# The first expert slot computed among the last attention tiles

## What is computed

```python
a = softmax(where(is_sink | in_window, q @ k.T / 8, -1e9));  x = a @ v      # (3072, 512)
expert_idx = argmax(x @ w_gate, axis=1);  gate_w = softmax(x @ w_gate)[expert_idx]
for e in range(8):
    mask = expert_idx == e
    out[mask] = gate_w[mask, None] * (maximum(x[mask] @ w1[e], 0) @ w2[e])  # 512 -> 1024 -> 512
h = out @ w_in                                                              # 512 -> 2048
result = (h - tanh(h)) @ w_out
```

## Time and profile before

| | us |
|---|---|
| median of 3 runs (lowest, highest) | 1080.17 (1079.96, 1080.34) |
| the profiled execution | 1080.2 |
| its span, first to last instruction | 1078.5 |
| PE busy | 1068.0 |
| DVE busy | 658.9 |
| POOL busy | 504.5 |
| ACT busy | 474.9 |

### The profile page before, as it was taken

How to read it: one execution, slowest core, us unless ns; L and a number is a source line. 1 busy time by engine, 2 the same in 40 slices (tenths; PEclk the granted TensorE clock), 3 DMA queues, 4 the chain that set the end, 5 groups by cost and what they waited for, 6 DMA issues and landing times.

```text
span 1078.5 us, 17085 instructions
## 1 busy us (share of the span) xinstructions
PE 1068.0 (99%) x5964; PEld 871.5 (81%) x5964; DVE 658.9 (61%) x1392; ACT 474.9 (44%) x1013; POOL 504.5 (47%) x521
## 2 busy tenths in 40 slices
PE   9999999999999999999999999999999999999997
PEld 6777776888888888888888888888888888888885
DVE  7898886443343434443388766666666666666664
ACT  7888884342152424541544333333333333333332
POOL 4375676634061707680463453335335335334433
PEclk9999999999999999999999999999999999999999
DMA  8656634625134425363321110101001011000001
GB/s 301 200 145 208 219 110 155 230 89 165 41 130 136 158 94 199 130 222 101 104 95 59 50 40 1 31 11 40 21 20 40 10 31 40 1 1 11 30 1 40
DMA packets 38204, 99.91 MB, mean 93 GB/s; under 512 B 8304, under 2 KB 8944, under 8 KB 33008
## 3 DMA queue, kind: packets, MB, share of 16 engines
q1 hardware_dynamic: 29248, 51.36, 15.3%
q0 software_dynamic: 8592, 47.31, 12.5%
q10 hardware_dynamic: 288, 0.26, 0.1%
HBM read 76.06 MB, written 22.86 MB: 92 GB/s over the span
## 4 chain that ended last, share of the span: by engine, by line
PE 92%; DVE 4%; issue 2%; ACT 1%; DMA 1%; POOL 0%; POOLq 0%; DVEq 0%; ACTq 0%
PE bank L800 24%; PE bank L808 23%; PE bank L740 15%; PE bank L726 14%; PE bank L492 3%; PE bank L530 2%; PE bank L732 2%; PE bank L507 2%; PE bank L471 1%; PE bank L701 1%; DVE prob L1099 1%; DVE probT L1115 1%; PE bank L784 1%; DMA sorted_x<-x_tok,dest 1%; PE bank L568 0%
## 5 line engine op out<-in xcount | busy, mean ns | idle before, releaser
L1564 POOL TENSOR_TENSOR weights<-raw,weights 128x1024 fp32r<-128x1024 f32 x70 | 166.7, 2401 | 190.9 <-ACT weights L869 188.8
L808 PE MATMUL bank<-weights,gT_hi 128*128 128x512 f32 x768 | 238.8, 392 | 0.3 <-DVE gT_lo L1431 0.3
L1673 POOL TENSOR_SCALAR ser<-ser 128x512 f32<-128x512 f32 x96 | 61.6, 642 | 281.1 <-DVE ser L1376 280.9
L800 PE MATMUL bank<-mT_hi,weights 128*128 128x512 f32 x768 | 189.8, 390 | 0.7 <-ACT mT_hi L1023 0.7
L800 PEld LDWEIGHTS bank<-mT_hi,weights 128*128 128x128 f32 x768 | 144.2, 188 | 30.7 <-ACT mT_hi L1023 0.9
L808 PEld LDWEIGHTS bank<-weights,gT_hi 128*128 128x128 f32 x768 | 142.7, 188 | 29.3 <-DVE gT_lo L1431 0.7
L808 PE MATMUL bank<-weights,gT_lo 128*128 128x512 f32 x384 | 149.8, 390 | 0.0
L740 PE MATMUL bank<-weights,hT_hi 128*128 128x512 f32 x464 | 148.7, 402 | 0.0
L1037 ACT ACTIVATE bank<-bank 128x512 f32<-128x512 f32 x96 | 55.9, 582 | 210.4 <-DVE ser L1407 210.4
L726 PE MATMUL bank<-weights,mT_hi 128*128 128x512 f32 x456 | 143.3, 395 | 0.0
L1675 POOL TENSOR_SCALAR sq<-sq 128x512 f32<-128x512 f32 x94 | 140.5, 1495 | 0.0
(11 more groups left out here) (163 smaller groups left out, 1639.4 us busy)
## 6 DMA issues: line engine op xcount, KB each, us to landing
raw<-w_all POOLq DMA_DIRECT2D x33, 1024.0 KB, 5.4
sorted_y<-ys SPq DMA_DIRECT2D x30, 261.0 KB, 2.8
xs<-sorted_x SPq DMA_DIRECT2D x29, 261.0 KB, 2.7
raw<-w_all SPq DMA_DIRECT2D x7, 1024.0 KB, 7.7
v_in<-vt SPq DMA_DIRECT2D x24, 256.0 KB, 4.2
kT<-kt SPq DMA_DIRECT2D x23, 264.0 KB, 3.6
qT<-qt SPq DMA_DIRECT2D x23, 256.0 KB, 4.6
raw<-sorted_y SPq DMA_DIRECT2D x20, 261.0 KB, 2.7
```

Source lines behind the costliest of these rows:

```text
L800: done = e.matmul(bank[HB[n % 3]][:, :], wt[:, f // 2, c, cols], x[:, c, :], start=(m == 0), stop=(m == 3 * CH - 1))
L808: done = e.matmul(bank[YB[i]][:, :], x[:, n % 3, rows], wt[:, f, :], start=(f == 0 and m == 0), stop=(f == GCH - 1 and m == 2))
L1564: e.tensor_tensor(lo, src, hi.bitcast(F32), ALU.subtract).then_inc(s_w_lo, 1)
L1673: e.tensor_scalar(row, row, SERIES_2, 1.0, ALU.mult, ALU.add).then_inc(s_ser, 1)
```

## The change

An early slot of expert 0 is added, made of the first 128 rows of its region as they stand after the scatters of sets 0 and 1 (the first twelve tiles). `sorted_x[0:128]` is set to zero at tile 3. At tile 22 SyncE loads the 128 rows and their gate fields. GpSimd multiplies them with the head factors, between its merges of pairs 1 and 2 in tile 21. In tile 22 TensorE turns them (a new entry in `turns`), ScalarE makes the high half, and VectorE the low half and the reciprocal of the gate. The slot's matmuls stand in the place of the `keep_warm` ones from tile 23 on, and of the 42 behind the counts. TensorE's waits for the next slot's rows come behind them.

If the counts of the first twelve tiles (`early_count`) show 128 rows or more for expert 0, `done_i` is 1, the loop of expert 0 makes one trip less and begins at row 128; else it begins at row 0 and its output overwrites that of the early slot. The body written out for expert 0 is gone: only its loop is left. All eight pieces of expert 0's weights are split during attention, and all four quarters of expert 1 are loaded in it. GpSimd splits nothing in the bridge; it waits for all scatters and then raises `x_turned` once, on which SyncE's first load waits. The three ranks of the last sets share one PSUM bank.

```diff
-    HI_IN, LO_IN, RAW_AT = (6, 6, 12, 12, 18, 18), (8, 9, 14, 15, 20, 21), (16, 18, 23)
+    HI_IN, LO_IN, RAW_AT = (4, 5, 6, 6, 12, 12, 18, 18), (5, 6, 8, 9, 14, 15, 20, 21), (16, 17, 18, 23)
+    EARLY = 1
@@ turns
+        if i == ALL - 2:
+            turns += [("slot", 0, (0,))]
@@ sync
+                if g == 3:
+                    e.wait_ge(c_zero, 4)
+                    e.dma_start(sorted_x[0:P, :], zeros[:, :]).then_inc(x_cleared, 16)
+                if g == ALL - 2:
+                    for b in range(EARLY + 1):
+                        e.wait_ge(scattered[b], 16 * SETS[b][1])
+                    e.dma_start(xs[:, :], sorted_x[0:P, :]).then_inc(x_loaded, 16)
+                    e.wait_ge(y_copied, 1)
+                    e.dma_start(ys[:, DM:META], sorted_x[0:P, DM:META]).then_inc(meta_in, 16)
...
             clear_tail(0)
-            for b in range(NSETS):
-                e.wait_ge(scattered[b], 16 * SETS[b][1])
-            e.wait_ge(tail_in[0], 16)
+            clear_tail(1)
...
-            e.reg_mov(r["x"], 0)
-            load_x()
-            clear_tail(1)
+            e.wait_ge(s_early_rows, 1)
             e.wait_ge(s_loops, 1)
-            e.wait_ge(s_offs, 1)
+            e.reg_load(r["x"], early_rows[0:1, 0:1])
+            e.reg_load(r["y"], early_rows[0:1, 0:1])
@@ tensor
+            def early_up(n, pieces):
+                products = [(xp, wt, c) for c in range(CH) for xp, wt in (
+                    (early_xT_hi, early_w1[0]), (early_xT_hi, early_w1[1]), (early_xT_lo, early_w1[0]))]
+                for m in pieces:
+                    xp, wt, c = products[m]
+                    done = e.matmul(bank[E_MH[n]][:, :], xp[:, c, :], wt[:, c, n * 512:(n + 1) * 512],
+                                    start=(m == 0), stop=(m == 3 * CH - 1), skip_group_check=True)
+                return done
...
+                if i == ALL - 2:
+                    early_turn_x()
...
                     e.wait_ge(s_masked, H * ALL)
-                    keep_warm(2)
+                    e.wait_ge(x_split, 1)
+                    e.wait_ge(s_w_lo, 8)
+                    early_up(0, range(0, 2))
...
-            keep_warm(5, bank[0])
+            early_up(0, range(8, 12)).then_inc(h_first, 1)
             rank(MULTI + 2)
...
-            keep_warm(42, bank[R_BANK])
+            early_up(1, range(0, 6))
+            e.wait_ge(relu_first, 1)
+            early_turn(0).then_inc(ht_first, 1)
+            early_up(1, range(6, 12)).then_inc(h_second, 1)
+            e.wait_ge(lo_first, 1)
+            e.wait_ge(s_x_copied, ALL)
+            early_down(range(0, 1))
+            e.wait_ge(relu_second, 1)
+            early_turn(1).then_inc(ht_second, 1)
+            early_down(range(1, 4))
+            e.wait_ge(lo_second, 1)
+            early_down(range(4, FCH)).then_inc(y_done, 1)
...
-            for _ in range(5):
+            for _ in range(14):
                 e.transpose(bank[R_BANK][:, 0:P], ident[:, :], ident[:, :])
-            e.wait_ge(s_loops, 1)
             for x in range(E):
-                slot_body(wbuf[x % 2], x)
+                if x:
+                    slot_body(wbuf[x % 2], x)
@@ scalar
+                if i == ALL - 2:
+                    e.wait_ge(early_turned, 1)
+                    e.activation(early_xT_hi[:, :, :], by_chunk(T_OF[turn_at["slot", 0, 0] % 2]), ACT.Copy).then_inc(x_hi, 1)
...
-            e.wait_ge(x_turned, 1)
+            e.wait_ge(s_offs, 1)
+            for b in range(NSETS):
+                e.wait_ge(scattered[b], 16 * SETS[b][1])
+            for y in range(0, 3):
+                split_hi(1, y)
+            e.wait_ge(x_turned, 2)
             e.activation(xT_hi, by_chunk(MT), ACT.Copy).then_inc(x_hi, 1)
+            e.activation(ys[:, 0:DM], bank[T_OF[1]][:, :], ACT.Copy, scale=early_gate[:, 1:2]).then_inc(y_copied, 1)
+            for y in range(3, 8):
+                split_hi(1, y)
@@ vector
                 at_once(routing)
+                if i == ALL - 2:
+                    bk = by_chunk(T_OF[turn_at["slot", 0, 0] % 2])
+                    e.wait_ge(x_hi, 1)
+                    e.tensor_tensor(early_xT_lo[:, :, :], bk, early_xT_hi[:, :, :].bitcast(F32), ALU.subtract).then_inc(x_split, 1)
+                    e.tensor_scalar(early_gate[:, 0:1], xs[:, DM:DM + 1], 1e-9, None, ALU.add).then_inc(gate_sum, 1)
+                    e.wait_ge(gate_sum, 1)
+                    e.reciprocal(early_gate[:, 1:2], early_gate[:, 0:1]).then_inc(gate_done, 1)
                 part(i, 0)
...
-            e.tensor_scalar(loops[:, :], count_i[:, :], 1.0, 1.0, ALU.max, ALU.subtract).then_inc(s_loops, 1)
+            e.scalar_tensor_tensor(out=loops[:, :], in0=count_i[:, :], scalar=1.0, in1=done_i[:, :], op0=ALU.max,
+                                   op1=ALU.subtract).then_inc(s_loops, 1)
@@ gpsimd
+                if g == SETS[EARLY + 1][0]:
+                    e.wait_ge(x_loaded, 16)
+                    e.wait_ge(meta_in, 16)
...
+                        if i == ALL - 3:
+                            e.wait_ge(x_loaded, 16)
+                            x = xs[:, 0:DM].rearrange("p (h d) -> p h d", d=D)
+                            e.tensor_tensor(x, x, xs[:, META:ROW].unsqueeze(2).broadcast_to([P, H, D]),
+                                            ALU.mult).then_inc(x_scaled, 1)
...
-            for y in range(len(LO_IN), 8):
-                split_lo(0, y)
+            for b in range(NSETS):
+                e.wait_ge(scattered[b], 16 * SETS[b][1])
+            e.wait_ge(gate_done, 1)
+            e.wait_ge(early_turned, 1)
+            e.sem_inc(x_turned, 1)
+            e.wait_ge(x_scaled, 2)
```

More of the change, by code:

```diff
@@ L461, in bank_of_turn @@
                         e.wait_ge(s_x_copied, wg_ + 1)
+                    elif was == "slot":
+                        e.wait_ge(x_split, 1)
                     elif part_on_act(wg_, pairs[-1]):
@@ L616, in rank, with early_turn_x, early_turn, early_down @@
                          start=False, stop=True, skip_group_check=True).then_inc(s_rank, 1)
+            E_MH, E_MHT, E_MY = (2, 3), (R_BANK, T_OF[0]), T_OF[1]
+            early_w = wbuf[0]
+            early_w1 = [early_w[:, a, 0:2 * QW].rearrange("p (c f) -> p c f", c=CH) for a in range(2)]
+            early_w2 = [early_w[:, a, 2 * QW:4 * QW].rearrange("p (c f) -> p c f", c=FCH) for a in range(2)]
+            def early_turn_x():
+                bk = bank_of_turn("slot", 0, 0)
+                e.wait_ge(x_scaled, 1)
+                for c in range(CH):
+                    done = e.transpose(bk[:, c * P:(c + 1) * P], xs[:, c * P:(c + 1) * P], ident[:, :])
+                done.then_inc(early_turned, 1)
+            def early_up(n, pieces):
[6 more added lines that the diff above has]
+                return done
+            def early_turn(n):
+                for c in range(CH):
+                    done = e.transpose(bank[E_MHT[n]][:, c * P:(c + 1) * P], early_hr[:, n, c * P:(c + 1) * P], ident[:, :])
+                return done
+            def early_down(chunks):
+                for c in chunks:
+                    for m, (xp, wt) in enumerate(((early_hT_hi, early_w2[0]), (early_hT_hi, early_w2[1]),
+                                                  (early_hT_lo, early_w2[0]))):
+                        done = e.matmul(bank[E_MY][:, :], xp[:, c, :], wt[:, c, :],
+                                        start=(c == 0 and m == 0), stop=(c == FCH - 1 and m == 2), skip_group_check=True)
+                return done
             e.wait_ge(c_ones, 1)
@@ L706, in slot_body @@
                 w2h, w2l = (w[:, a, 2 * QW:4 * QW].rearrange("p (c f) -> p c f", c=FCH) for a in range(2))
-                def first_up():
-                    products = [(xT_hi, wt, c) for c in range(CH) for wt in (w1h, w1l)] + [(xT_lo, w1h, c) for c in range(CH)]
-                    for m, (xp, wt, c) in enumerate(products):
-                        if m < 2 * CH and m % 2 == 0:
-                            e.wait_ge(s_w_lo, c + 1)
-                        if m == 2 * CH:
-                            e.wait_ge(x_split, r["this"])
-                        done = e.matmul(bank[MH[0]][:, :], xp[:, c, :], wt[:, c, 0:512],
-                                        start=(m == 0), stop=(m == 3 * CH - 1))
-                    return done
                 def up(n, chunks):
@@ L967, in scalar @@
             x_copy(ALL - 1)
-            for y in range(len(HI_IN), 8):
-                split_hi(0, y)
+            e.wait_ge(ht_first, 1)
+            e.activation(early_hT_hi[:, 0:CH, :], by_chunk(R_BANK), ACT.Copy).then_inc(hi_first, 1)
+            e.wait_ge(ht_second, 1)
+            e.activation(early_hT_hi[:, CH:FCH, :], by_chunk(T_OF[0]), ACT.Copy).then_inc(hi_second, 1)
             r = {n: e.alloc_register(f"act_{n}") for n in ("this", "next", "trips")}
             e.wait_ge(s_loops, 1)
-            e.reg_mov(r["this"], 1)
-            e.reg_mov(r["next"], 2)
+            e.reg_mov(r["this"], 2)
```

(10 more changed lines are left out.)

142 lines of the change are left out of this document (82 added, 60 removed).

## The result

The changed kernel takes **1071.97 us** (median; 1071.83 to 1072.5), the kernel before 1080.26 beside it: a ratio of 0.9924 (95% interval 0.9906 to 0.9941), 8.3 us less. The forecast was 1071.5. The profiled execution took 1071.8, with a span of 1070.1 against 1078.5: 8.4 less.

A forecast was written before the change was run, and what follows sets the result against it. TensorE's queue, 92% of the chain, was taken as the bound. Gain 11.25 - 1.7 (tile 21) - 0.6 (tile 22) - 0.15 (restart) - 0.1 (ranks' wait) = 8.7 us: 1071.5 us, range 1069.4 to 1073.6.

The forecast's parts named there:

- Rivals 3 and 4: 3: TensorE's clock falls in the bridge, 1079.7, chance 0.03; 4: early slot does not count, 1083.8, chance 0.03.
- The bridge: TensorE behind the counts: early slot takes what 42 matmuls took, plus 0.3 us stall, ending at 180.2 us.
- The restart: From early slot to next slot: 0.6 + 1.43 us, next slot at 182.25; the rows' path costs 0.15 more.
- rival 2: At the restart, late rows or ScalarE's weight copies become the bound: plus 0.7 to 2 us, 1072.8, chance 0.2.
- ScalarE's five weight copies: Before the first `hi_first`: 4.9 us against 4.8 available; cost zero, up to 1 us if both copy groups slip.
- Tile 22: VectorE's added subtraction and two gate operations before `part(22, 0)` partly fill its idle time: cost 0.6 us (0 to 1.1).
- Tile 21: GpSimd's 1.3 us multiply: VectorE's cast is held over it and merge 2, cost 1.7 us (0 to 2.8).
- rival 1: In tile 21 VectorE's cast is let in between GpSimd instructions, so the 1.7 falls away: 1069.8, chance 0.2.
- The forecast's bound of 0.5 us for tiles 4 to 20: In attention: the forecast is wrong if anything in these tiles moves by over 0.5 us.
- The slots behind and the second layer only move: After the restart: later slots and the second layer shift in time, with no cost of their own.
- the earlier split and the moved load: Tiles 4 and 5, and tile 23's 1 MB load on SyncE: each costed at 0, the ScalarE copy up to 0.2.
- 11.25: Gain before costs in us: second slot at 193.50 in the old kernel, next slot at 182.25 in the new.

The follow-up runs named there:

- the loop run: The changed kernel with the bar for a finished early slot above any count, so expert 0's loop makes four trips: 1086.71 us, kernel before 1083.76.
- the run with the adds: The changed kernel with VectorE's casts of destinations and tally, in all sets, written as adds of a zero: 1071.65 us.
- the first experiment: The kernel before with only the changed kernel's tiles for the first expert's weight splits and raw loads: ratio 1.0011, 1.2 us slower.

## Why the prediction was right

The median came 0.5 us above the forecast, in its range. Its mechanism, one slot taken out of the loops into the bridge, is shown by the loop run (12.30 us). Rivals 3 and 4 did not come: the clock was 1.00, and 28 slots are in the loops. The sum is another matter: two terms were too dear (tiles 21 and 22), one was missing (the close) and some smaller ones too cheap, and they nearly cancel.

- **The bridge.** In the old kernel's time (minus 1.27) the early slot ends at 181.35 + 0.23 (one matmul) - 1.27 = 180.31; 180.2 was said. The stall of 0.3 was put ahead of `early_down`, and the chain shows it there (175.45: three matmuls take 0.96 and not 0.68).
- **The restart.** 2.35 us from the early slot's end to the first looped slot, against 0.6 + 1.43 = 2.03, and 0.15 more for the rows. The rows did bind, by 0.17 (181.58 to 181.75); VectorE waits 2.95 us for them. The load is issued at 178.13, 1.85 after the old 176.28, of which 1.27 is the attention's. ScalarE's five weight copies end 0.30 before `hi_first` is due: no stall, as costed. Of rival 2, which said 0.7 to 2 us, there is 0.17: its mechanism is there, its size is not.
- **Tile 22.** 0.37 us for the 0.6 said, by the mechanism said: the subtraction fills VectorE's wait. What it costs depends on how long that wait was. Before `part(22, 0)` VectorE idled 0.38 in the trace before, and 0.67 to 0.69 in the three variants of the kernel before, in which tile 22 took 7.50 to 7.52 us; the changed kernel takes 7.59. Against these the edit costs 0.1.
- **Tile 21: the mis-sized term.** 1.7 said, 0.22 to 0.36 measured. Both halves were wrong: the multiply takes 1.06 us and not 1.3, and VectorE was let in before it. This is rival 1, to which a chance of 0.2 was given; the 1.7 was the sum's largest error. The Trainium skill, "SBUF — State Buffer", section "Who interferes with whom", has the first to issue hold the port for its whole instruction; tile 21 agrees (0.47 us), while the 5.36 us of a cast over a scatter and two splits does not. I had drawn a rule from one row between two splits and applied it to two merges and a multiply.
- **Tiles 19 and 20.** 0.43 us that nobody costed: 13.86 together, against 13.43 before (127.20 to 140.63). The edits don't bring it: three runs of the old attention have 13.42 to 13.43, and so have eight variants of the changed one, with and without the multiply; only the changed kernel's own trace and the run with the adds (13.76) show it. In both an operation of VectorE with two SBUF inputs meets a merge and takes 0.76 or 0.77 us instead of 0.20 (at 136.81 before, 137.01 after). The forecast's bound of 0.5 us for tiles 4 to 20 just holds (tile 21 starts 0.47 late).
- **The missing term.** "The slots behind and the second layer only move" held to 0.14 us (9.57 at the first looped slot, 9.43 at the last matmul). The 1.05 at GpSimd's close is outside of what I read: I followed the chain by engine and never the stores behind the last matmul. The part of the change costed at 0, the earlier split and the moved load, is enough to bring it, as the first experiment shows; giving the load back does not take it away.

Sum by what was measured: 11.25 - 0.41 (bridge and restart) - 1.27 (attention) - 0.14 - 1.05 = 8.4 us. By the forecast: 8.7. With the multiply sized rightly and nothing else, it would have been 1070.2, further off: the forecast's closeness is partly luck.

## What to carry to other kernels

Work that TensorE does only to bridge a wait is room for real work, and the gain is the length of what leaves the loop; what is left to check is whether the data of that work is ready a stage ahead. A lock between VectorE and GpSimd that was read off one pair of instructions holds for that kind of pair only: look for the nearest kind in the trace, and keep both ends of the range as rivals. Read the chain behind the last matmul as carefully as the part that is changed: here a microsecond went there with an edit of GpSimd's program hundreds of us earlier. And compare a single tile between two single traces only when more traces of either kernel agree on it.

## What the runs showed of the hardware

- GpSimd's close is one of two lengths, 4.3 or 6.1 us from its start to the end of the span, with a last gap between stores of 1.95 or 1.27 us; 1.05 us apart in sum. The three traces with GpSimd's old program have the short one, the eleven with an edited program the long one; the number of its DMA instructions (80 to 85), of its packets (8448 to 8608) and the queue of the 1 MB load make no difference.
- VectorE was held for 5.36 us, whatever its operation (an add, a `tensor_scalar`, a cast of 3 columns), over a scatter and two splits of 4.66 us together, and for 3.15 to 3.20 us in each of six scalings that started under the first of two splits in the old trace. Between merges of 0.73 us and a multiply of 1.06 it was let in each time, twice in each of the eight traces that have the multiply there (0.31 to 0.48 and 0.65 or 0.66 us).
- A multiply of 128x512 in fp32 on GpSimd takes 1.05 to 1.06 us.
- After TensorE idled for 2.4 to 2.75 us at the end of attention (eight traces), its granted clock was 0.50 for 3.4 us (two of them) or 6.8 us (six). With idle times of at most 0.18 us there (the other six traces) it stayed at 1.00.
